# A mask table built with min and max, a weight piece moved from VectorE to POOL, and a last output step finished group by group

## The reference

```python
rel = pos[:, None] - pos[None, :]
is_global = pos[None, :] < int(n_global)                  # 8
is_local = (rel >= 0) & (rel < int(n_local))              # 96
keep = is_global | is_local
dist = np.where(is_global & ~is_local, float(n_local), np.abs(rel).astype(np.float32))
scores = scale * np.matmul(q, k.transpose(0, 1, 3, 2)) - slopes[:, None, None] * dist
scores = np.where(keep, scores, -1e9)                     # then softmax, then @ v -> x (1536 x 512)
h = x @ w_in;  g = np.maximum(h, 0) + alpha * np.minimum(h, 0);  x = g @ w_out      # layer 1, d_ff 2048
h = x @ w_in;  P = a0 + a1*h + a2*h**2 + a3*h**3;  Q = 1 + abs(b0)*abs(h) + abs(b1)*h**2
out = (P / (Q + 1e-6)) @ w_out                                                      # layer 2, d_ff 2048
```

## Time and profile before

| what | value |
|---|---|
| median of three runs | 655.75 us |
| the profiled execution | 655.03 us, of which the span is 653.3 us |
| PE busy | 630.9 us (97%) |
| DVE / ACT / POOL busy | 466.6 / 311.7 / 283.9 us |
| chain that ended last | PE 86%, DVE 3%, POOL 2%, ACT 2%, issue 2%, DMA 1% |

### The profile page before, as it was taken

The page is one execution under the profiler, slowest core; times in us unless marked ns, Lnnn a source line. Parts: engine busy times, 40 slices in busy tenths (PEclk is TensorE's granted clock), DMA queues, the critical chain, the costliest instruction groups (busy, mean ns, idle before and its releaser), DMA issues.

```text
span 653.3 us, 9458 instructions
## 1 busy us (share of the span) xinstructions
PE 630.9 (97%) x3048; PEld 505.6 (77%) x3048; DVE 466.6 (71%) x763; ACT 311.7 (48%) x664; POOL 283.9 (43%) x225
## 2 busy tenths in 40 slices
PE   4989999999999999999999998999999999999996
PEld 3657777777877777778888887888888888888884
DVE  7867776665476666646555559988859988699884
ACT  5862332423233333322111175766667766687662
POOL 4568560000000000001444478777758777487772
PEclk9999999999999999999999999999999999999999
DMA  5664421211011111010222210000010000100001
GB/s 150 198 200 125 134 62 29 54 32 30 0 28 33 51 28 38 0 46 19 97 96 98 96 65 0 2 0 2 1 65 0 0 0 0 53 13 0 1 1 68
DMA packets 38932, 31.27 MB, mean 48 GB/s; under 512 B 9008, under 2 KB 33264, under 8 KB 38896
## 3 DMA queue, kind: packets, MB, share of 16 engines
q1 hardware_dynamic: 38896, 30.83, 15.3%
HBM read 27.67 MB, written 3.15 MB: 47 GB/s over the span
## 4 chain that ended last, share of the span: by engine, by line
PE 86%; DVE 3%; POOL 2%; ACT 2%; issue 2%; DMA 1%; SPq 0%; DVEq 0%; POOLq 0%; ACTq 0%
PE ps_h L564 28%; PE ps_y L592 19%; PE ps_y L594 18%; PE ps_s L564 5%; PE ps_o L564 5%; PE ps_s L516 4%; PE ps_o L537 3%; PE ps_o L526 2%; PE ps_y L483 1%; POOL numer L1256 1%; DMA kT<-in_k 1%; POOL denom L1254 1%; POOL numer L1259 1%; PE ps_o L507 1%; DVE ps_o L1036 1%
## 5 line engine op out<-in xcount | busy, mean ns | idle before, releaser
L564 PE MATMUL ps_h<-xy_hi,win_hi 128*128 (+1 forms) x288 | 118.5, 412 | 0.7 <-DVE xy_lo L954 0.7
L1247 POOL TENSOR_TENSOR win_lo<-stage,win_hi 128x1024 fp32r<-128x1024 f32 x8 | 19.2, 2404 | 230.0 <-DVE win_hi L1012 230.0
L564 PE MATMUL ps_h<-xy_lo,win_hi 128*128 (+1 forms) x288 | 112.6, 391 | 0.0
L564 PE MATMUL ps_h<-xy_hi,win_lo 128*128 (+1 forms) x288 | 112.4, 390 | 0.0
L726 ACT ACTIVATE g_hi<-g 128x512 fp32r<-128x512 f32 x48 | 30.3, 631 | 134.7 <-PE ps_y L592 125.0
L1254 POOL TENSOR_TENSOR denom<-denom,q_abs 128x512 f32<-128x512 f32 x48 | 63.1, 1315 | 69.4 <-ACT denom L746 69.4
L1036 DVE RECIPROCAL ps_h<-denom 128x512 f32<-128x512 f32 x24 | 80.6, 3360 | 17.4 <-POOL denom L1254 16.9
L592 PE MATMUL ps_y<-g_hi,wout_hi 128*128 128x512 f32 x192 | 80.9, 421 | 0.0
L1029 DVE TENSOR_TENSOR g_lo<-g,g_hi 128x512 fp32r<-128x512 f32 x48 | 33.7, 701 | 64.9 <-ACT g_hi L726 64.9
L592 PE MATMUL ps_y<-g_hi,wout_lo 128*128 128x512 f32 x192 | 75.2, 392 | 0.0
L594 PE MATMUL ps_y<-wout_hi,g_hi 128*128 128x512 f32 x192 | 74.8, 390 | 0.0
(11 more groups left out here) (146 smaller groups left out, 1267.3 us busy)
## 6 DMA issues: line engine op xcount, KB each, us to landing
stage<-in_w_in SPq DMA_DIRECT2D x8, 512.0 KB, 3.3
stage<-in_w_out SPq DMA_DIRECT2D x8, 512.0 KB, 3.2
qT<-in_q SPq DMA_DIRECT2D x48, 64.0 KB, 2.4
kT<-in_k SPq DMA_DIRECT2D x24, 128.0 KB, 2.4
vv<-in_v SPq DMA_DIRECT2D x24, 128.0 KB, 2.2
out<-xy_raw SPq DMA_DIRECT2D x12, 256.0 KB, 2.2
xy_raw<-in_w_in SPq DMA_DIRECT2D x4, 512.0 KB, 4.9
xy_raw<-in_w_out SPq DMA_DIRECT2D x4, 512.0 KB, 4.4
```

Of the source, the lines that this page charges most:

```text
L564: mm = pe.matmul(ps_h_at(layer, m), w[:, kc, cut], x[:, blk, kc, :], start=(kc == 0 and n == 0), stop=(kc == KC - 1 and n == 2))
```

## The change

1. The distance table is written with fewer instructions. "Not allowed" is a very large distance (`FAR`), so the table is a maximum of distances, with a minimum against the global columns. `later_keep` is gone, `later_distances` has two small instructions, and it moves from step 2 to step 1. POOL waits for the whole table (`dist_ready` at 4) before its first weight piece.
2. The last weight piece of layer 2 goes from DVE at the border of the layers to POOL within block 0 of layer 2: two rounding copies behind m = 6 and 7, four subtractions of 128 x 256 behind m = 8 to 11. POOL's hardware loop over the first two blocks becomes straight code.
3. The last output step finishes its groups one after the other, so that a group's three matmuls are nearer together, and the copies wait group by group.

```diff
@@ PE, output: the last m of the last block
+                lo_at = 2 * KC
+                if after is None and m == MC - 1:
+                    lo_at = 4
+                    passes = passes[0:4] + passes[8:10] + passes[4:6] + passes[10:11] + passes[6:8] + passes[11:12]
...
-                    if after is None and m == MC - 1 and n == 2 * KC + 1:
-                        mm.then_inc(y_half_done, 1)
+                    if after is None and m == MC - 1 and g is g_lo and j < KC - 1:
+                        mm.then_inc(y_part_done, 1)
@@ ACT
-            act.wait_ge(dist_ready, 1)
+            act.wait_ge(dist_ready, 2)
...
-                    act.wait_ge(dist_ready, 3)
+                    act.wait_ge(dist_ready, 4)
...
             for j in range(0, KC, 2):
-                act.wait_ge(*((y_done, 2 * BLOCKS * MC) if j else (y_half_done, 1)))
+                act.wait_ge(y_part_done, j + 1)
@@ DVE, first_distances and later_distances
-                chained(dve.tensor_scalar(keep, rel, 0.0, None, ALU.is_ge))
+                chained(dve.tensor_scalar(ahead, rel, 0.0, FAR, ALU.is_lt, ALU.mult))
+                chained(dve.tensor_tensor(ahead, ahead, rel, ALU.max))
                 dve.wait_ge(n_in, 16)
                 chained(dve.tensor_copy(nn[:, :], nn_i[:, :, 0]))
...
+                chained(dve.tensor_scalar(far_glob, near, ng, FAR, ALU.is_ge, ALU.mult))
+                chained(dve.tensor_scalar(far_local, rel, nl, FAR, ALU.is_ge, ALU.mult))
+                dve.tensor_tensor(even, far_local, ahead, ALU.max).then_inc(dist_ready, 1)
                 dve.wait_ge(dist_ready, 1)
+                dve.scalar_tensor_tensor(out=dist[:, D_FIRST:D_FIRST + P], in0=far_glob, scalar=nl, in1=dist[:, D_EVEN:D_EVEN + P],
+                                         op0=ALU.max, op1=ALU.min).then_inc(dist_ready, 1)
-            def later_keep():
...
             def later_distances():
...
+                cut = slice(D_EVEN + P, D_EVEN + P + GLOB)
+                dve.tensor_scalar(dist[:, cut], far_glob[:, 0:GLOB], nn[:, 1:2], None, ALU.max).then_inc(dist_ready, 1)
                 dve.wait_ge(dist_ready, 3)
+                dve.tensor_copy(dist[:, D_ODD:D_ODD + P], dist[:, D_EVEN + P:D_EVEN + 2 * P]).then_inc(dist_ready, 1)
...
                     if arg == 1:
-                        later_keep()
+                        later_distances()
                         denominator(0, 0)
                     if arg:
                         inverse(0, arg - 1)
-                    if arg == 2:
-                        later_distances()
@@ DVE, border of the layers and end
-                elif what == "done":
-                    weights(MC - 1)
...
-                    dve.tensor_tensor(lo, staged(stage2, MC - 1, kind), hi.bitcast(F32), ALU.subtract).then_inc(w_ready, 1)
...
-                dve.wait_ge(*((y_done, 2 * BLOCKS * MC) if j > 1 else (y_half_done, 1)))
+                dve.wait_ge(*((y_done, 2 * BLOCKS * MC) if j == KC - 1 else (y_part_done, j + 1)))
@@ POOL
+            pool.wait_ge(dist_ready, 4)
             for n in range(2 * PIECES):
...
-            with pool.Fori(0, BLOCKS - 1) as blk:
+            for blk in range(BLOCKS - 1):
                 for what, arg in block_events(1, False, "block"):
                     if what == "g":
                         gate2(blk + arg // MC, arg % MC)
+                    if blk == 0 and what == "g" and arg in (6, 7):
+                        row = arg - 6
+                        pool.wait_ge(w_in[1][last % len(stage2)], 16 * (last // len(stage2) + 1))
+                        pool.wait_ge(y_done, MC * BLOCKS)
+                        pool.tensor_copy(last_hi[:, row, :], last_raw[:, row, :]).then_inc(last_hi_ready, 1)
+                    if blk == 0 and what == "g" and arg in (8, 9, 10, 11):
+                        row, cut = (arg - 8) // 2, slice(arg % 2 * HALF, arg % 2 * HALF + HALF)
+                        pool.wait_ge(last_hi_ready, row + 1)
+                        ins = pool.tensor_tensor(last_lo[:, row, cut], last_raw[:, row, cut], last_hi.bitcast(F32)[:, row, cut],
+                                                 ALU.subtract)
+                        if arg == 11:
+                            ins.then_inc(w_ready, 1)
```

More of the change, by code:

```diff
@@ L154, in build_program @@
         spare = xy_raw_lo[:, 1].rearrange("p c t -> p (c t)")
-        rel, keep, charge, fill = (spare[:, 2 * P * i:2 * P * (i + 1)] for i in range(4))
-        near, glob, glob_keep, glob_charge, glob_fill = (spare[:, P * i:P * (i + 1)] for i in range(8, 13))
+        rel, ahead, far_local = (spare[:, 2 * P * i:2 * P * (i + 1)] for i in range(3))
+        near, far_glob = (spare[:, P * i:P * (i + 1)] for i in range(6, 8))
         def psum(name, shape):
@@ L584, in output @@
                         pe.wait_ge(y_read, (blk + BLOCKS * layer) * KC + (j + 1))
-                    if n == 2 * KC and layer == 1:
+                    if n == lo_at and layer == 1:
                         pe.wait_ge(g2_ready, MC * blk + (m + 1))
-                    elif n == 2 * KC:
+                    elif n == lo_at:
                         pe.wait_ge(g_ready, c + 1)
-                    flags = dict(start=(m == 0 and n < 2 * KC and n % 2 == 0), stop=(m == MC - 1 and n >= 2 * KC))
+                    flags = dict(start=(m == 0 and n < 2 * KC and n % 2 == 0), stop=(m == MC - 1 and g is g_lo))
                     cut = slice(j * P, (j + 1) * P)
@@ L887, in first_distances @@
-                chained(dve.scalar_tensor_tensor(out=keep[:, own], in0=rel[:, own], scalar=nl, in1=keep[:, own],
-                                                 op0=ALU.is_lt, op1=ALU.mult))
-                chained(dve.tensor_tensor(charge[:, own], rel[:, own], keep[:, own], ALU.mult))
-                chained(dve.tensor_scalar(glob, near, ng, None, ALU.is_lt))
-                chained(dve.scalar_tensor_tensor(out=glob_fill, in0=keep[:, 0:P], scalar=0.5, in1=glob,
-                                                 op0=ALU.is_lt, op1=ALU.mult))
@@ L894, in first_distances @@
-                chained(dve.tensor_tensor(glob_keep, keep[:, 0:P], glob_fill, ALU.add))
-                chained(dve.scalar_tensor_tensor(out=glob_charge, in0=glob_fill, scalar=nl, in1=charge[:, 0:P],
-                                                 op0=ALU.mult, op1=ALU.add))
-                chained(dve.tensor_scalar(glob_fill, glob_keep, -FAR, FAR, ALU.mult, ALU.add))
-                dve.tensor_tensor(dist[:, D_FIRST:D_FIRST + P], glob_charge, glob_fill, ALU.add).then_inc(dist_ready, 1)
-                dve.wait_ge(dist_ready, 1)
@@ L1288, in _ @@
                     weights(1, order2, MC - 2)
-            with pool.Fori(0, BLOCKS - 1) as blk:
+            last = 2 * PIECES - 1
+            last_hi, last_lo = piece_views(*order2[last])
+            last_raw = staged(stage2, last, order2[last][0])
+            for blk in range(BLOCKS - 1):
                 for what, arg in block_events(1, False, "block"):
```

19 lines of the change are left out of this document (3 added, 16 removed).

## The result

| | before | after |
|---|---|---|
| median of six runs | 656.01 us (653.59 to 656.98) | 647.81 us (646.88 to 649.04) |
| ratio, 95% interval | | 0.9895 (0.9877 to 0.9913) |
| the profiled execution, its span | 655.03, 653.3 us | 649.04, 647.2 us |

The ratio is 6.9 us of 655.75, with an interval from 5.7 to 8.1. The kernel became faster, by more than the 0.5% that a measurement can tell. The forecast was 648.5 us. Two executions of more than twice the usual time, one of 2020 us of the kernel before and one of 1614 us of e10, are left out of the ratios.

The account below looks back on a forecast made before the run. TensorE, busy in 97% of the span, was taken as the bound. Start 2.1, middle 3.8 and end 1.0 sum to 6.9 us off 655.03, so 648.1; 648.5 us was taken, range 646.0 to 651.2.

Parts of the forecast that it names:

- The first shift, the norm and step 4's scores: Start: shift at 6.4 to 6.5, bound by score records; step 1's norm at 9.9; step 4's scores about 12.0.
- It costs nothing: Start: POOL's new wait costs 0 us, as the table is ready at about 8.3, before the first piece's data at 9.2.
- The 2.1 us of the start: Start: the new table's gain for TensorE, taken as 2.1 us, with ends of 0.6 and 3.6.
- the walk through steps 2 and 3: Start: following turn, exponentials, bias and copy, TensorE's turn of step 3 comes 2.0 us earlier, ACT's copy 2.3.
- TensorE is fast sooner: Rival, start and end: earlier fast pace and no store's pause, 1.6 us more gain, 646.9 us; chance 0.17.
- The rival on loads: Rival, start: DMA and SP's queue set the loads' pace, only 0.6 of 2.1 us stays, 649.9 us; chance 0.16.
- The middle, 3.8 us: Layer border: with two instructions off DVE, TensorE's `g_lo` wait and slow clock go, 2.38 + 1.44 us; bounds 1.9 and 4.2.
- the second term: Middle: the 12 matmuls from 408.24 to 412.40 take 4.16 us instead of 2.72 at the lower clock, 1.44 us.
- The end, 1.0 us: Last output step: first copy 1.13 us earlier, last store issued about 1.0 earlier; 1.0 us gained, at least 0.3.
- The stores bound the end: End: four store issues take 3.20 us, the third 1.53; if that repeats, the last is issued about 1.0 us earlier.
- The middle's wait was replaced: Rival, middle: ACT or POOL is as late as DVE was, half of 3.8 us is lost, 650.4 us; chance 0.06.
- POOL's pieces were not locked out: Rival, middle: new POOL instructions wait for whole reciprocals, 3 us lost each time, slower at 657.5 us; chance 0.03.

Follow-up runs that it names:

- e10: The changed kernel with six extra TensorE matmuls on zeros ahead of the first scores; ratio to the kernel before 0.9887.
- e6: The changed kernel without POOL's wait for the distance table; ratio to the kernel before 0.9904.
- e5: The kernel before, old table instructions kept, with one added wait of POOL for the whole table; ratio 0.9938, 4.1 us faster.
- e1: The kernel before with only the new distance table, POOL's wait for it and DVE's new order; ratio 0.9949, 3.3 us faster.
- e3: The kernel before with only the last output step and its copies done group by group; ratio 0.9995, 0.3 us faster.
- e4: The changed kernel with the last output step, its copies and waits as before; ratio to the kernel before 0.9914, 5.6 us faster.
- e8: The changed kernel with the last stores of groups 0 and 2 issued by ACT instead of SP; ratio to the kernel before 0.9897.
- e2: The kernel before with only the last weight piece moved from DVE to POOL; ratio 0.9962, 2.5 us faster.
- e7: The changed kernel with POOL's last weight piece done in one go behind m = 6, not in six instructions; ratio to the kernel before 0.9902.

## Why the prediction was right, and where its sizes were off

648.5 us was forecast, 647.8 measured. The start and the middle did what was said; the last step did it as far as the first copy, while its gain in time isn't shown. Point by point:

**The first shift, the norm and step 4's scores.** Forecast at 6.4 to 6.5, 9.9 and 12.0; they came at 6.51, 9.74 and 11.85. The bound named for each held.

**"It costs nothing" on POOL's wait** is true of the changed kernel (e6). But it is half the story: where line 913 "lost 2 us" to POOL, the forecast put the whole value on the instructions that go. e5 keeps them all and gains as much. The Trainium skill, "SBUF — State Buffer", section "Who interferes with whom", says that the port pair that VectorE and GpSimd share is an exclusive lock. The trace agrees: 2.36 us beside POOL, 0.29 without it.

**The 2.1 us of the start.** The hidden mark is at 48.43 on average in the three profiles with the old start, and at 45.69 in nine with the new (all but e10): 2.7 us, and 3.3 timed (2.0 to 4.7). 2.1 is inside, a little low. The step that missed is the walk through steps 2 and 3 at "the pace of today". The pace comes at 18.3 on average in the three profiles with the old start and at 14.2 in the nine with the new. Where the pace comes at the same time, in e1 (18.1) and e3 (18.2), the marks are only 0.98 apart. Where it comes at 9.4 to 13.3 instead of 19.0 (e4, e8), 4.0 us are gained. So the term of 2.1 is too large at an equal pace, as far as one pair of profiles can tell, and an earlier pace, which it left to a rival, makes up for it. In the changed kernel's own profile the rival "TensorE is fast sooner" came true and step 5's scores went in 1.03 us instead of 1.66; its other half, the store's pause, did not go. The forecast held that the granted clock doesn't show this change; the view doesn't, but the trace does, as told in the last section. The rival on loads did not come: waits for k in the profile are 0.23 and 0.74 us, against 1.24 before.

**"All marks behind 20 us earlier by 2".** The mark at 58.87 was earlier by 2.45, the hidden one by 3.58. The difference between the two, POOL's pieces beside DVE in block 0, was in no term. It looks like the collision that the forecast had seen in line 913, at a place where it did not look, because these pieces were untouched: DVE's two operations grow by 0.58 and 0.57 us, and one POOL subtraction of this form takes 0.74. The pieces lie elsewhere against DVE's work because the start is earlier.

**The middle, 3.8 us.** In the trace it is exact: from the mark near 182 us to T0, 459.37 us before and 455.57 after, 3.80 less. But e2 alone gives 2.5 (1.4 to 3.5), below it; in its own profile the stretch takes 455.91 us, as `g_lo` is waited for 0.52 us once, right ahead of T0, instead of 0.19. The failed step is "the second term is the lower clock; it goes only with the stall", counted at its full 1.44 us. That presumes that every execution of before has it. It doesn't: e5 has the same stall, and no lower clock behind it. One microsecond of e5, then the same of e1, which has the same stall 0.03 us later:

```profile
408.00:409.00 1.00, 1.00 (x6) 0.82 (x5) 1.00 (x1) 1.00 (x2) 0.21 (x1) 1.00 0.00 0
```

```profile
408.00:409.00 1.00, 1.00 (x4) 0.81 (x3) 1.00 (x1) 1.00 (x2) 0.19 (x1) 0.50 0.00 0
```

The clock column reads 1.00 in the one (2.4 GHz) and 0.50 in the other (1.2 GHz). From mark to T0 e5 takes 457.77 us, 1.6 less than before. The executions show the same in their mean granted clock: of 50 of the kernel before, run beside the experiments, 30 stand at 0.996 or below, with a median of 655.7 us, and 20 at 0.997 or above, with 654.2. Of 58 executions without the stall at the border (all kernels but before, e1, e3, e5), 4 are below 0.997; of the 24 of e1, e3 and e5, which keep the stall, 10 are. The mean clock is a rough sign, but the two medians lie 1.5 us apart, which is the size of the term. By this estimate the second term is 1.44 x 30/50 = 0.9 us on average, and the middle 2.38 + 0.9 = 3.2 us, inside e2's interval.

**The end, 1.0 us.** The first copy is earlier by 1.14, as forecast (1.13), and the last group is complete no later. But the changed kernel's tail is 0.5 us longer. The step that failed is "The stores bound the end", by which an earlier last issue ends the span as much earlier. In the changed kernel the pause came one store sooner, so that it held up three stores instead of two; the last issue was still 0.62 us earlier behind T0, but its landing took 1.2 us longer. In e3 it was 2.28 us earlier, for 0.5 us of tail, and in e8 2.30 us earlier, for a tail of 9.0 as before. So the end follows the landing and not the issue. In time the last step is worth 0.3 us by e3 (-0.7 to 1.3) and 1.2 by e4; neither the 1.0 nor the "at least 0.3" of the forecast is shown or ruled out. The tails, 9.4 us on average in the old order and 9.3 in the new, speak for little.

**The rivals that did not come.** The middle's wait was replaced by none. POOL's pieces were not locked out: the changed kernel's four subtractions of 128 x 256, from 422.73 to 439.79, lie wholly beside reciprocals of 3.36 us and take 0.74 us each, the least of the earlier trace rows. The 2.41 us subtraction of e7 lies beside none, so it says nothing here. And of POOL's three instructions per `m` only two run beside the reciprocal, before as well (1.28 us from 633.53 and 1.29 from 634.90, beside the one from 633.60): that of the earlier trace rows makes its input.

**The sum.** Start 2.1, in truth 2.7 to 3.3; middle 3.8, in truth about 3.2 on average; end 1.0, measured as 0.3 and as 1.2. The first two errors are of opposite signs and cancel, and the ratio's 6.9 us is the forecast's sum to the digit. That is luck in part.

## What to carry to other kernels

When one operation takes many times what its neighbours of the same size do, look at what lies beside it on the engine that shares its way to memory. A wait that keeps the two apart may be worth as much as writing the work anew, and shorter instructions on the other engine may make the rest of the program less a matter of chance. Before the cost of a lower clock is counted in full, see in how many executions it is there: one profile shows one of two outcomes. And an earlier issue of the last stores is worth something only if the end waits for the issue and not for the landing.

## What the runs showed of the hardware

- The same stall of TensorE (1.9 us) is followed by some 3 us at the lower clock in some executions and not in others, e1 and e5 above. About three in five executions of the kernel before had it, by their mean clock.
- In the start, matmuls of one form run at two durations (1.91 to 2.08 and 1.03 us for a step's scores), and the change from one to the other comes anywhere from 9.4 to 18.1 us in kernels with the same order of work there. Each us later puts the hidden mark some 0.3 us later (an estimate, a line through the nine profiles with the new start). The column of the granted clock reads 1.00 throughout, before the change too, but only because nothing is recorded: the trace's list of granted clocks has its first entry, at 1.00, at 18.72 us in the kernel before and at 13.46 in the changed one. In all 14 profiles it begins between 0.60 us ahead of the first short duration and 0.03 behind it. So the short durations are those of the full clock (2.4 GHz), and the column can't be used before that entry.
- Four store issues on SP take 2.05 to 2.12 us in e2 to e5, and 2.96 to 4.04 in the other eight profiles with all four there, one issue in them being a long one. The wait for the landing behind them is 3.7 to 4.1 us in the first group and 2.2 to 3.8 in the second: much of the pause comes back there, and the tail is 9.4 us on average in the first group and 9.3 in the second.
